# Second FFN's first matrix in 15 products instead of 18, with the sums of its weights made in the first FFN

## The reference

```
x = attention(q, k, v, f_logit)                  # [3072, 384]
x = ((x @ w_a) * (x @ w_b)) @ w_out              # first FFN, 1536 wide
p = domain_probs / domain_probs.sum(-1)
for e in range(4):                               # second FFN, 4 experts, 1024 wide
    out += p[:, e:e+1] * (relu(x @ w1[e]) @ w2[e])
```

## Time and profile before

| | us |
|---|---|
| median of 3 runs (1369.57 to 1369.71) | 1369.68 |
| the profiled execution's own time | 1369.83 |
| its span in the profile | 1368.1 |
| PE busy, share of the span | 1354.0, 99% |
| DVE, ACT, POOL busy | 791.4, 613.2, 590.8 |
| chain that ended last: PE's share | 96% |
| granted TensorE clock, mean | 0.997 |

### The profile page before, as it was taken

How to read it: one execution, slowest core, us unless ns; L and a number is a source line. 1 busy time by engine, 2 the same in 40 slices (tenths; PEclk the granted TensorE clock), 3 DMA queues, 4 the chain that set the end, 5 groups by cost and what they waited for, 6 DMA issues and landing times.

```text
span 1368.1 us, 23021 instructions
## 1 busy us (share of the span) xinstructions
PE 1354.0 (99%) x8355; PEld 1328.7 (97%) x8355; DVE 791.4 (58%) x1556; ACT 613.2 (45%) x1183; POOL 590.8 (43%) x595
## 2 busy tenths in 40 slices
PE   8999999999999999999999999999999999999999
PEld 7899999999999999999999999999999999999999
DVE  8775555556542222246666667666667666666665
ACT  5544433433422322245555455554445554445452
POOL 4542221212210301046666555666566665555551
PEclk9999999999999999999999999999999999999999
DMA  7542322323200000012222231222322122322111
GB/s 170 151 121 51 65 53 57 66 49 62 53 11 27 0 1 1 12 35 70 70 70 70 70 97 60 64 71 70 101 73 61 58 69 70 104 70 70 59 59 59
DMA packets 69315, 87.28 MB, mean 64 GB/s; under 512 B 5712, under 2 KB 67664, under 8 KB 69200
## 3 DMA queue, kind: packets, MB, share of 16 engines
q1 hardware_dynamic: 69200, 85.79, 22.9%
HBM read 76.33 MB, written 4.72 MB: 59 GB/s over the span
## 4 chain that ended last, share of the span: by engine, by line
PE 96%; DVE 1%; issue 0%; ACT 0%; ACTq 0%; DVEq 0%
PE bank L1296 12%; PE bank L1298 11%; PE bank L1297 11%; PE bank L1443 10%; PE bank L1445 10%; PE bank L1444 10%; PE bank L1384 9%; PE bank L1386 9%; PE bank L1385 9%; PE bank L1261 2%; PE bank L1291 2%; PE bank L1284 1%; PE bank L1270 1%; PE bank L1246 1%; PE bank L1347 0%
## 5 line engine op out<-in xcount | busy, mean ns | idle before, releaser
L892 POOL TENSOR_TENSOR wu_lo<-raw,wu_hi 128x768 fp32r<-128x768 f32 x64 | 118.6, 1853 | 331.8 <-ACT wu_hi L703 331.8
L1162 DVE SCALAR_TENSOR_TENSOR xt<-bank,pn,xt 128x384 f32<-128x384 f32 x360 | 214.2, 616 | 77.1 <-PE bank L1445 77.1
L1443 PE MATMUL bank<-wd_hi,h_hi 128*128 128x384 f32 x768 | 257.1, 335 | 1.1 <-DVE xt L1159 1.1
L722 ACT ACTIVATE h<-bank 128x384 f32<-128x384 f32 x256 | 125.9, 493 | 294.8 <-PE bank L1386 292.7
L1444 PE MATMUL bank<-wd_lo,h_hi 128*128 128x384 f32 x768 | 256.9, 334 | 0.0
L1445 PE MATMUL bank<-wd_hi,h_lo 128*128 128x384 f32 x768 | 256.8, 334 | 0.0
L1144 DVE TENSOR_TENSOR h<-h,bank 128x384 f32<-128x384 f32 x256 | 141.5, 553 | 180.8 <-PE bank L1386 153.9
L1384 PE MATMUL bank<-x_hi,wu_hi 128*128 128x384 f32 x704 | 236.2, 336 | 0.7 <-ACT h L722 0.7
L1386 PE MATMUL bank<-x_lo,wu_hi 128*128 128x384 f32 x704 | 236.3, 336 | 0.0
L1385 PE MATMUL bank<-x_hi,wu_lo 128*128 128x384 f32 x704 | 236.1, 335 | 0.0
L1296 PE MATMUL bank<-xs_hi,wab_hi 128*128 128x384 f32 x576 | 199.3, 346 | 0.4 <-issue 0.4
(11 more groups left out here) (102 smaller groups left out, 2206.0 us busy)
## 6 DMA issues: line engine op xcount, KB each, us to landing
raw<-w SPq DMA_DIRECT2D x128, 384.0 KB, 3.1
unit<-fkq SPq DMA_DIRECT2D x62, 216.0 KB, 4.3
v_in<-v_chunks SPq DMA_DIRECT2D x32, 144.0 KB, 4.0
out<-xt SPq DMA_DIRECT2D x24, 192.0 KB, 1.9
xt<-ystage SPq DMA_DIRECT2D x48, 72.0 KB, 2.2
raw<-wa SPq DMA_DIRECT2D x6, 384.0 KB, 3.8
raw<-wb SPq DMA_DIRECT2D x6, 384.0 KB, 3.4
raw<-wo SPq DMA_DIRECT2D x6, 384.0 KB, 3.6
```

What stands on the lines that cost most here:

```text
L1162: eng.scalar_tensor_tensor(out=acc(b, t), in0=d, scalar=w, in1=acc(b, t), op0=ALU.mult, op1=ALU.add).then_inc(s_acc, 1)
L1443: eng.matmul(o, hh, w_hi, start=(f == 0), stop=False)
```

## The change

- A group is now three hidden tiles (FG = 3), counted through all experts: 32 tiles are NQ = 10 groups of three and a last one of two, GP = 11 groups a pair, 44 in all. Groups 2 and 5 of a pair reach over two experts; `down_2` makes their six output tiles in two parts each, and `weigh` takes both.
- For a full group 3 f x 3 k x 2 blocks takes 15 products (R) in four chains, instead of 18. They are on 11 sums of x tiles and 6 plain ones (NX = 17, NXS = 11), and on 15 combinations of w1 tiles. The last group is done plainly (`up_last`, 12 products).
- The 15 combinations are made once for each of the ten groups, in the first FFN, from j = SUMS_AT = 182 on at a pace of 7 steps a group: `load_w1(q)` into `raw`, 16 POOL instructions (`w_sum`) and 4 ACT copies (`w_copy`) into the one buffer `w_s`, `store_sums(q)` to a DRAM tensor `wsum`. In the second FFN `load_wu` reads them back in three pieces into the same `w_s`, and ACT and POOL split them, for each of the four pairs.
- PE's order is part n of up_2(g), then output tile n of group g-1. The output tiles have two banks, the chains six.
- There is one set of x operands. Those of the next pair are made by ACT and POOL at the end of the pair: six after group 9, eight after group 10, three at the start of the next pair (order X_NEXT); eight of the sums by DVE in groups 4 to 7, three after group 10. In a pair's first group each product waits for its own x operand (position in X_NEXT).
- The first FFN's weights are laid out by tile, so that the new buffers can be put over tiles that are done with. `add` has ten steps a group (four before), `copy` five (four before, for two tiles).

The core of the diff (small helpers, the other sums and the order lists of DVE and ACT in a full group are left out):

```diff
-    FP = FT2 // 2
-    GP = E * FP
+    FG = 3
+    NQ = E * FT2 // FG
+    LAST = E * FT2 - FG * NQ
+    GP = NQ + 1
...
+    R = 15
+    MADE = (8, 14, 1, 13, 9, 3, 2, 7, 12, 4, 11, 5, 10, 6, 0)
+    CHAINS = (0, 1, 2, 3, 0, 1, 2, 3, 0, 2, 3, 0, 2, 3, 0)
+    WP = R // 3
+    B10, B21 = 15, 16
+    X_TILE = {13: (1, 1), 3: (0, 1), 4: (2, 0), 0: (0, 0), B10: (1, 0), B21: (2, 1)}
+    X_FIRST = (1, 2, 5, 9, 7, 6, 8, 14, 12, 11, 10, 13, 3, 4, 0, B10, B21)
+    X_NEXT = (8, 14, 1, 9, 2, 7, 12, 11, 5, 10, 6, 13, 3, B21, 4, 0, B10)
+    NX = len(X_FIRST)
+    NXS = 11
+    PLAIN_X = ((0, B10, 4), (3, 13, B21))
+    H_ORDER = (1, 2, 4, 5, 3, 0)
+    H_LAST = (1, 3, 0, 2)
+    T_ORDER = (3, 4, 5, 0, 1, 2)
...
-    X2_AT = CMIN_AT + 20
-    U2_AT = 3 * FT1 * (NB1 - 1) + 4
+    SUMS_AT, SUMS_PACE = CMIN_AT + 12, 7
+    WU_AT, WD_AT = 3 * FT1 * (NB1 - 1) + 20, 3 * FT1 * (NB1 - 1) + 29
+    def x2_at(n):
+        return SUMS_AT + 2 + 5 * n if n < 9 else 3 * FT1 * (NB1 - 1) + 2 + 2 * (n - 9)
...
+        def x2_free(eng, b, o):
+            n = x_slot(o)
             if b == 0:
+                if n < 9:
+                    attention_done(eng)
+                else:
+                    eng.wait_ge(s_upb, FT1 * (NB1 - 1) + max(0, (n - 10) // 2))
+            elif o not in X_TILE:
+                eng.wait_ge(s_step, steps(GP * b - 1) - R + MADE.index(o) + 1)
             else:
+                eng.wait_ge(s_step, steps(GP * b - 1) + (2 if X_TILE[o][1] else 4))
...
+            def load_w1(q):
+                if q == 0:
                     eng.wait_ge(s_whi, R1)
                     eng.wait_ge(s_wlo, R1)
                 else:
+                    eng.wait_ge(s_ws, 16 * q)
+                    eng.wait_ge(s_wc, 4 * q)
+                dst = raw.rearrange("p a n -> p (a n)")[:, 0:KT * FG * 128].rearrange("p (k f) -> p k f", k=KT)
+                for e, fs in shares(q):
+                    f0 = (f_tiles(q)[fs[0]] - e * FT2) * 128
+                    width = 128 * len(fs)
+                    eng.dma_start(dst[:, :, 128 * fs[0]:128 * fs[0] + width],
+                                  w1[e, :, f0:f0 + width].rearrange("(k p) f -> p k f", p=128)).then_inc(s_wr, 16)
+            def store_sums(q):
+                eng.wait_ge(s_ws, 16 * (q + 1))
+                eng.wait_ge(s_wc, 4 * (q + 1))
+                eng.dma_start(wsum[q], w_s[:, :, :]).then_inc(s_wst, 16)
+            def load_wu(g, n):
                 if g == 0:
+                    eng.wait_ge(s_wst, 16 * NQ)
                 else:
+                    eng.wait_ge(s_uhi, 3 * (g - 1) + n + 1)
+                    eng.wait_ge(s_ulo, 3 * (g - 1) + n + 1)
+                b, q = group(g)
+                if q < NQ:
+                    src = wsum[q, :, n * WP:(n + 1) * WP, :]
+                else:
+                    f0 = (FT2 - LAST) * 128
+                    src = w1[E - 1, n * 128:(n + 1) * 128, f0:].rearrange("p (f n) -> p f n", n=128)
+                eng.dma_start(wu_raw(g, n), src).then_inc(s_wu[n], 16)
+            def load_wd(g):
+                if g == 0:
+                    eng.wait_ge(s_ws, 16 * NQ)
...
+                if j == SUMS_AT - 4:
                     load_w1(0)
+                for q in range(NQ):
+                    if j == SUMS_AT + SUMS_PACE * (q + 1):
+                        store_sums(q)
+                        if q + 1 < NQ:
+                            load_w1(q + 1)
+                if j == WU_AT - 8:
+                    load_wd(0)
+                    for n in range(3):
+                        load_wu(0, n)
+                if j == WU_AT + 8:
+                    for n in range(3):
+                        load_wu(1, n)
             for g in range(G):
                 if g + 2 < G:
+                    for n in range(3):
+                        load_wu(g + 2, n)
+                if g + 1 < G:
+                    load_wd(g + 1)
+                if g % GP == 1 and g > GP:
                     store_out(g // GP - 1)
...
+            def w_copy(q, n):
+                r, f, k = ((14, 1, 2), (12, 2, 1), (5, 2, 0), (6, 1, 0))[n]
+                eng.wait_ge(s_wr, w_loads(q))
+                eng.wait_ge(s_wst, 16 * q) if q else attention_done(eng)
+                eng.activation(w_s[:, MADE.index(r), :], w1_raw(f, k), ACT.Copy).then_inc(s_wc, 1)
...
+                for q in range(NQ):
+                    for n in range(4):
+                        if j == SUMS_AT + SUMS_PACE * q + n:
+                            w_copy(q, n)
                 for n in range(NX):
+                    if j == x2_at(n):
                         x2_round(0, n)
...
+                if g % GP == 0 and g:
+                    for n in range(NX - 3, NX):
+                        x2_round(g // GP, n)
...
+                else:
+                    if g + 1 < G:
+                        up_round(g + 1, 0)
+                    last_round(g, 0)
+                    if g + 1 < G:
+                        up_round(g + 1, 1)
+                    last_round(g, 1)
+                    if g + 1 < G:
+                        up_round(g + 1, 2)
+                    down_round(g, 0)
+                    last_round(g, 2)
+                    down_round(g, 1)
+                    last_round(g, 3)
+                if g // GP + 1 < NP and g % GP == NQ - 1:
+                    for n in range(6):
+                        x2_round(g // GP + 1, n)
+                if g // GP + 1 < NP and g % GP == NQ:
...
+            def w_sum(q, n):
+                if n == 0:
+                    eng.wait_ge(s_wr, w_loads(q))
+                    eng.wait_ge(s_wst, 16 * q) if q else attention_done(eng)
+                def a(f, k):
+                    return w1_raw(f, k)
+                def s(r):
+                    return w_s[:, MADE.index(r), :]
+                if n == 0:
+                    eng.tensor_tensor(s(1), a(1, 2), a(0, 2), ALU.subtract).then_inc(s_ws, 1)
...
+                elif n == 14:
+                    eng.wait_ge(s_ws, 16 * q + 13)
+                    eng.tensor_tensor(s(0), s(7), a(0, 0), ALU.add).then_inc(s_ws, 1)
                 else:
+                    eng.wait_ge(s_ws, 16 * q + 15)
+                    eng.tensor_tensor(s(0), s(0), a(2, 0), ALU.add).then_inc(s_ws, 1)
...
+                for q in range(NQ):
+                    for n in range(16):
+                        if j == SUMS_AT + SUMS_PACE * q + n * 6 // 16:
+                            w_sum(q, n)
                 for n in range(NX):
+                    if j == x2_at(n):
                         x2_rest(0, n)
...
+            def x2_sum(b, n):
                 if n == 0:
                     x2_ready(eng, b)
                     if b == 0:
+                        attention_done(eng)
+                ring = NXT if b else 2
+                if n >= ring:
+                    eng.wait_ge(s_x2lo, NX * b + n - ring + 1)
+                elif b:
+                    eng.wait_ge(s_x2lo, NX * (b - 1) + NXS)
+                (b00, b01), (b10, b11), (b20, b21) = ((x_tile(2 * b, k), x_tile(2 * b + 1, k)) for k in range(KT))
+                o = x_order(b)[n]
+                to = x_sum_buffer(b, n)[:, :]
+                if o in (2, 5, 7, 6):
+                    ahead = {2: 1, 5: 2, 7: 9, 6: 7}[o]
+                    eng.wait_ge(s_x2t, NXS * b + x_order(b).index(ahead) + 1)
+                    that = x2_from(b, ahead)
...
+                else:
+                    weigh(g - 1, 0)
+                    weigh(g - 1, 1)
+                    last_rest(g, 0)
+                    weigh(g - 1, 2)
+                    last_rest(g, 1)
+                    weigh(g - 1, 3)
+                    weigh(g - 1, 4)
+                    last_rest(g, 2)
+                    weigh(g - 1, 5)
+                    last_rest(g, 3)
+                if g // GP + 1 < NP and 4 <= g % GP < 8:
                     for n in range(2):
+                        x2_sum(g // GP + 1, 2 * (g % GP - 4) + n)
+                if g // GP + 1 < NP and g % GP == NQ:
+                    for n in range(NXT, NXS):
+                        x2_sum(g // GP + 1, n)
...
+            def product(g, n, start):
+                b, q = group(g)
+                o = MADE[n]
+                if n % WP == 0:
+                    eng.wait_ge(s_uhi, 3 * g + n // WP + 1)
+                    eng.wait_ge(s_ulo, 3 * g + n // WP + 1)
+                if q == 0:
+                    eng.wait_ge(s_x2hi, x_made(b, o) if b else NX)
+                    eng.wait_ge(s_x2lo, x_made(b, o) if b else NX)
...
                 if part == 0:
+                    chain_free(g, 0)
+                    product(g, 0, True)
+                    chain_free(g, 1)
+                    product(g, 1, True)
+                    chain_free(g, 2)
+                    product(g, 2, True)
+                    chain_free(g, 3)
+                    product(g, 3, True)
+                elif part == 1:
+                    eng.wait_ge(s_add, adds(g) + 1)
+                    product(g, 4, False)
```

(66 more changed lines are left out.)

695 lines of the change are left out of this document (388 added, 307 removed).

## The result

The changed kernel takes **1408.78 us**, the median of 4 runs (1407.65 to 1409.52), beside 1369.62 (1369.07 to 1369.71) for the kernel before. The ratio is 1.0286, with a 95% interval of 1.0268 to 1.0304: slower by 2.9%. The profiled execution took 1407.65 us, its span is 1405.9.

What follows compares the result with a forecast made beforehand. PE's instruction count was taken as the bound, waits reaching PE adding whole. 1369.8 - 29.1 + 32.8 + 1.7 + 20.4 + 3 = 1398.6 for the profiled execution, forecast 1398 us, range 1362 to 1416.

Steps and rivals of the forecast that it cites:

- the two mechanisms: Serial sums and transfers hold ACT, then PE, in the first FFN; late x operands stop PE at three pair boundaries.
- What is removed: Second FFN: 168 fewer matmuls on w1 at 0.1734 us each, 29.1 us less.
- The sums in the first FFN: Sums, then store and load, in series, nine transfers 54.9 us: PE +32.8 us late, plus +1.7 for the clock.
- The round: First FFN: one round of sums, store and load takes 13.9 us where the pace of seven steps allows 10.97.
- the rival of covered rounds: First FFN rounds fit the pace, transfer 3.5 us or less, only the boundaries wait: 1364 us, chance 0.10.
- DVE beside the sums: First FFN: two-input DVE instructions lengthen POOL's work, 0.7 us a round, 6 us over nine rounds (bounds 0 and 15).
- The case of 15 us: First FFN: three DVE instructions a round each block POOL for their whole 0.56 us; 15 us instead of 6, result 1407.
- The boundaries: Three pair boundaries: PE waits 5.1 us for operand 13 behind POOL's subtractions, plus 1.7 of clock; +20.4 us (bounds 9 and 30).
- The start of the second FFN: Group 0 has only down_1(95) between its products, so PE waits for DVE and ACT: net +3 us (bounds 0 and 6).
- Groups at "nothing": Full second-FFN groups hide DVE, ACT, POOL and loads: no cost (bounds 0 and 0.3 us a group), two-expert groups included.
- Only the sums wait: Rival: boundary operands come in time, only the first FFN's sums cost: 1378 us, chance 0.14.
- More waits: Rival: transfer of 7.5 us and full lock, 12.6 and 9 more, or late adds: 1410 to 1420 us, chance 0.09.

Runs made afterwards that it cites:

- the second parts shortened: The best version with the second weighing of 48 two-expert output tiles done on 8 columns instead of 384: 1351.10 us.
- each partial repair: Changed kernel with only a new order of the x operands, 1402.42 us, or only DVE's late sums moved earlier, 1402.78 us.
- the best version: Changed kernel with sum rounds at a pace of ten steps, new x operand order and DVE's three late sums spread singly: 1354.96 us, ratio 0.9893.
- the run of order and sums together: Changed kernel at its own pace of seven, with new x operand order and DVE's three late sums spread singly in a pair's last group: 1393.85 us.
- the run with the earlier sums: Changed kernel with DVE's last three x sums behind the second weighing of a pair's last group, old operand order: 1402.78 us.

## Why the prediction was right, step by step

The sign, the two mechanisms and their places held; the time was 10.8 us higher than 1398.

- **What is removed, 29.1 us.** The second FFN now runs from PE's first product at 633.07 to 1405.9, 772.8 us, where it was 774.7. With 29.1 less, 27.2 came in its place. By the lengths of the groups on PE these are 20.5 us at the boundaries, 1.8 net at the start, 4.3 in and behind the groups over two experts, and 0.6 that stay open.
- **The sums in the first FFN, +34.5 predicted, +39.7 measured** (633.07 for 593.38). By dates: round 0 ended at 437.24 (436.6 predicted). The eight phases of sums took 71.2 us together (70.4 predicted). The nine transfers took 59.0 us, not 54.9: this is the mis-sized term. The first turn took 7.42 us, the two whose load is made of two transfers 6.66 and 6.54, one with a slow issue 6.68, and the other five 6.33 to 6.37. One of these five, in windows:

```profile
469.83:470.60 0.77, 0.77 (x7) 0.77 (x6) 0.00 (x0) 0.00 (x0) 0.77 (x1) 1.00 0.00 0
470.60:472.10 1.50, 0.97 (x6) 0.65 (x4) 0.00 (x0) 0.00 (x0) 0.19 (x1) 1.00 1.06 410
472.10:474.10 2.00, 0.00 (x0) 0.00 (x0) 0.00 (x0) 0.00 (x0) 0.00 (x0) 1.00 0.90 214
474.10:475.60 1.50, 0.00 (x0) 0.00 (x0) 0.00 (x0) 0.00 (x0) 0.00 (x0) 1.00 0.94 353
```

  The bytes start some 0.85 us after the last sum, where I had 1.27, but need 5.0 us and not 4.3: the rate falls to 214 GB/s for 2 us in the middle, about where the store's bytes end and the load's begin. The load goes out 0.42 to 0.45 us behind the store in all nine turns; whether that makes the dip, no run shows. Together 0.6 + 0.8 + 4.1 = 5.5 later at round 9. The runs without transfers and with a double store show that the series of sums and transfer is the cause, not POOL's load.
- **The round.** The prediction's own terms make a round of 14.9 us (6.1 of transfer and 70.4 / 8 of sums), not the 13.9 that it states beside them; its dates and its +32.8 are by the right one. Measured are 15.35. By these terms the rival of covered rounds would have needed a transfer of 2.6 us, not 3.5.
- **DVE beside the sums, 6 us predicted.** 21 sums of rounds 1 to 9 took 0.77 to 0.83 for 0.46, 6.7 us in all: that term was right. The case of 15 us took each of three meetings a round at DVE's whole 0.56. Each cost 0.32, and the traces still agree with the exclusive lock of the Trainium skill's page "SBUF — State Buffer" (section "SBUF: two separate sides"): in all 21 cases the sum ends 0.3 us after the DVE instruction beside it, so it had waited for its end, and only part of DVE's time was left to wait for. What was too high was the price of a meeting, not the rule.
- **The boundaries, +20.4 predicted, +20.5 measured** (20.61, 21.64 and 20.65 us for the first groups of a pair, where those without a wait take 14.13). The wait is 4.84 us where I had 5.1, for the operand, by the engines and in the order that the step named. The clock costs some 2.0 us each where I had 1.7, as the second boundary has 6.8 us at half speed and not 3.4.
- **The start of the second FFN, +3 predicted.** The waits are 1.1, 0.7, 0.6 and 0.3, 2.7 us, where before had 1.8 in this stage, of which I had taken off only 0.7: +0.9. By the time of the first 100 matmuls it is +1.8 (21.51 us for 19.74). Both are inside its bounds of 0 and 6.
- **Groups at "nothing".** True for the full groups of one expert: with the second parts shortened 60 us hold 346 and 347 matmuls, 0.173 us each, the cadence of the earlier trace rows. For the two-expert groups it was wrong: in the changed kernel PE takes 17.61 to 17.69 us for each of the eight, 17.22 for the others behind a pair's start, and 17.51 to 17.53 for the one behind in three pairs, where the prediction had DVE's lateness end in that group's slack. I had weighed DVE's sum of work against the length of the group, and named the two tile banks as what would hold PE next, but not charged them. A tile of two parts needs both banks within one slot of 1.56 us, with two weighings of some 0.62 us each behind it, and no average shows that.
- **The rivals.** "The rounds are covered" would have needed a far shorter transfer than the 6.3 to 7.4 us that it took. "Only the sums wait" needed a boundary without a wait. "More waits", 1410 to 1420, came close to the measured time for partly the wrong reason: neither a transfer of 7.5 us nor 9 us more beside DVE is there. The sum of 1398.6 was 9.0 us under the profiled execution: 5.2 in the first FFN, 4.3 for the two-expert groups, 0.1 at the boundaries and 0.6 that stay open, less 1.2 at the start. The median is 1.1 us above that execution. So no large errors cancelled; inside the transfer term a start 0.4 us earlier than assumed hid part of the slower bytes.

## What to carry to other kernels

A waiting instruction put into an in-order program makes everything queued behind it wait; give it a date no earlier than work and transfer in series allow (here ten steps for seven, 40.7 us), before anything is made faster. When a wait is taken away at a handover, follow every engine's program there, not the one that was seen to wait: each partial repair here won 4 or 5 of the 20.5 us and moved the wait, both together won 11.4 and 13.8. Look also at POOL's program beside DVE's splits: a row of its subtractions without a gap held one of them for 5.1 us. And price a group with a double result by its slots, not by its sums.

## What was not expected of the hardware

The same waits were followed by different clocks. After the three waits of 4.84 us the clock stayed at 1.2 GHz for 3.4, 6.8 and 3.4 us; with the pace of ten, for 6.8, 3.4 and 6.8. Two short waits of 1.0 us, 2.3 us apart, left it at 2.4 GHz at all three places of the best version, but in the run of order and sums together the same two were followed by 3.4 us at half speed at one of the three, and so in the run with the shortened part. And the wait of 3.7 us in the run with the earlier sums was followed by none. Windows of the run of order and sums together, then around that wait of 3.7 us:

```profile
1206.00:1211.50 5.50, 3.53 (x19) 2.93 (x18) 5.50 (x8) 1.84 (x5) 4.45 (x4) 1.00 0.38 119
1211.60:1215.00 3.40, 3.40 (x12) 3.40 (x11) 1.81 (x4) 0.91 (x3) 1.57 (x1) 0.50 0.59 177
```

```profile
828.90:832.50 3.60, 0.00 (x0) 0.00 (x0) 3.60 (x4) 0.00 (x0) 2.21 (x2) 1.00 0.63 192
832.60:842.60 10.00, 10.00 (x58) 10.00 (x59) 8.68 (x18) 5.20 (x11) 4.26 (x4) 1.00 0.27 88
```

So the length of one wait did not decide here whether the clock falls.

A POOL sum of 128x128 in SBUF took 0.77 to 0.83 us instead of 0.46 when it met an instruction of DVE, never a value in between in the 21 cases of rounds 1 to 9. The other way round it is not bounded so: one DVE split of 0.56 us took 5.66 while POOL's subtractions followed one another. And a 1.57 MB exchange through DRAM in one queue, store then load, cost 6.3 to 6.7 us from the last sum to the first in eight of nine turns, 7.4 in the first.
